# Local attention scores through DRAM bands, values weighed by rows of tokens on GpSimd and VectorE, from the third half-batch on

## The reference

```python
B, H, S, D = 4, 8, 576, 64; factor = 4; scale = 1 / sqrt(D)
# q, k, v pooled by the mean of 4 tokens: softmax attention over 144, each row repeated 4 times
out_up = repeat(softmax(scale * q_d @ k_d.T) @ v_d, factor)
# local attention: only keys with |i - j| < 4, so 7 of them
scores = where(abs(i - j) < factor, scale * q @ k.T, -1e9)
out_local = softmax(scores) @ v
x = (out_up + out_local) as (2304 tokens, 512)
h = x @ w1_in;  x = (h * sigmoid(h)) @ w1_out            # 512 -> 2048 -> 512
r = relu(x @ w2_in);  out = (s * r * r + b) @ w2_out     # 512 -> 2048 -> 512
```

## Time and profile before

| | |
|---|---|
| median of 3 runs | 978.97 us |
| profiled execution | 980.76 us, span 978.8 us |
| granted TensorE clock, mean | 0.997 |
| matmuls on the chain of waits | 93% of the span |
| VectorE, ScalarE, GpSimd busy | 46%, 38%, 36% |
| first layer, tile to tile | 69.3 us; 51.5 us for the last, without attention |

### The profile page before, as it was taken

How to read it: one execution, slowest core, us unless ns; L and a number is a source line. 1 busy time by engine, 2 the same in 40 slices (tenths; PEclk the granted TensorE clock), 3 DMA queues, 4 the chain that set the end, 5 groups by cost and what they waited for, 6 DMA issues and landing times.

```text
span 978.8 us, 17604 instructions
## 1 busy us (share of the span) xinstructions
PE 968.6 (99%) x6449; PEld 900.8 (92%) x6449; DVE 450.0 (46%) x1105; ACT 370.0 (38%) x1143; POOL 351.8 (36%) x366
## 2 busy tenths in 40 slices
PE   8999999999999999999999999999999999999998
PEld 8899999999999999999999998888888888888897
DVE  5577556565465555555554654224222322322232
...
DMA packets 71189, 60.64 MB, mean 62 GB/s; under 512 B 24272, under 2 KB 58576, under 8 KB 71120
## 3 DMA queue, kind: packets, MB, share of 16 engines
...
...
## 4 chain that ended last, share of the span: by engine, by line
PE 93%; DVE 4%; ACT 1%; issue 1%; DMA 1%; SPq 0%; POOL 0%; ACTq 0%; DVEq 0%
PE pH L599 20%; PE pY L614 20%; PE pH L541 19%; PE pY L546 18%; PE pO L484 4%; PE pS L441 3%; PE pO L480 2%; PE pO L457 2%; PE pS L444 2%; DVE w_in_hl L237 1%; PE pO L460 1%; DVE w_out_hl L237 1%; ACT w_in_hl L638 1%; DVE act L871 1%; PE pY L557 1%
## 5 line engine op out<-in xcount | busy, mean ns | idle before, releaser
L237 POOL TENSOR_TENSOR g_hl<-act,g_hl 128x288 fp32r<-128x288 f32 (+2 forms) x208 | 199.6, 960 | 602.4 <-ACT g_hl L638 602.4
L546 PE MATMUL pY<-g_hl,w_out_hl 128*128 128x288 f32 x1536 | 246.5, 300 | 0.4 <-POOL g_hl L237 0.4
L541 PE MATMUL pH<-x_hl,w_in_hl 128*128 128x288 f32 x1518 | 238.2, 301 | 2.8 <-issue 1.8
L541 PEld LDWEIGHTS pH<-x_hl,w_in_hl 128*128 128x128 f32 x1518 | 212.2, 190 | 3.2 <-issue 3.2
L546 PEld LDWEIGHTS pY<-g_hl,w_out_hl 128*128 128x128 f32 x1536 | 213.0, 188 | 0.6 <-POOL g_hl L237 0.6
L599 PE MATMUL pH<-x_hl,w_in_hl 128*128 128x512 f32 (+1 forms) x960 | 208.4, 368 | 0.0
L614 PE MATMUL pY<-w_out_hl,g_hl 128*128 128x512 f32 x864 | 207.8, 390 | 0.0
L599 PEld LDWEIGHTS pH<-x_hl,w_in_hl 128*128 128x128 f32 x960 | 169.0, 188 | 31.0
L614 PEld LDWEIGHTS pY<-w_out_hl,g_hl 128*128 128x128 f32 x864 | 161.2, 188 | 33.1 <-POOL g_hl L237 0.3
L638 ACT ACTIVATE g_hl<-act 128x288 fp32r<-128x288 f32 (+2 forms) x208 | 104.0, 500 | 213.8 <-DVE act L871 110.1
L992 DVE TENSOR_TENSOR act<-act 128x512 f32<-128x512 f32 (+1 forms) x80 | 55.5, 694 | 270.6 <-ACT act L793 270.6
...
## 6 DMA issues: line engine op xcount, KB each, us to landing
...
```

What stands on the lines that cost most here:

```text
L237: eng.tensor_tensor(lo, full, hi.bitcast(F32), ALU.subtract).then_inc(signal, 1)
L541: last = pe.matmul(pH[:, f % 2, 0:T1], w_in[:, wp, c, f * P:(f + 1) * P], x1[:, par, mp, c, :], start=c + n == 0, stop=c == C - 1 and n == 2)
L546: last = pe.matmul(pY[:, c, 0:T1], w_out[:, wp, f, c * P:(c + 1) * P], g_hl[:, f % RING, mp, 0:T1], start=f + n == 0, stop=f == NF - 1 and ...
```

## The change

Units 0 to 15 are done as before. From unit 16 on (`by_rows`), TensorE makes the scores as before, but ScalarE copies the three local blocks to SBUF in place of the exponentials, and SyncE stores them in DRAM (`store_band`) and reads only the 7 keys of each token back (`read_band`), so that a partition holds two heads of a block of 9 tokens: 4 pairs of heads by 32 blocks are 128 partitions. When a half's eight heads are there, one softmax is taken over the half, on VectorE and ScalarE: `row_shift`, `row_exps`, `row_normalise` (126 numbers a partition). For each row i of the 9 tokens a product of 896 numbers (2 heads, 7 keys, 64 features) is made by GpSimd, or by VectorE for i = 2, 5, 8 (`weigh`); VectorE sums over the keys (`sum_row`). TensorE transposes the rows in groups of three (`turn`), ScalarE moves them to `x_rows` (`place`), VectorE adds the pooled part (`x_add`), ScalarE rounds (`x_round`) and GpSimd subtracts (`x_low`). The values come in four loads a half (`load_windows`). The local transposes, local attends, masks and copies of these units go away.

To have the scores in time, a unit's scores are made seven units ahead: tile 1 works units 1 to 14 of its half and the next, two in each of slots 0 to 5; tiles 2 to 5 one a slot; tile 6 has one unit left. A loop pass is now tiles 2 and 3, then 4 and 5. Small edits: 20 short memsets for an edge mask ahead of `first_sums` on VectorE, a larger identity, buffers laid out anew, and the second layer's first weight loads behind the wait on `x1_ready`.

```diff
+TB = 9
+NB = HALF // TB
+NR = 2 * POOL - 1
+ROWS = TB + NR - 1
+BAND = KW + 1
+EDGES = 3
+NEW = 2 * H
+LEAD = 7
+UNITS = [(u + LEAD,) for u in range(H)]
+FIRST_UNITS = [(1, 2), (3, 4), (5, 6), (7, 8), (9, 10), (11, 12), (13,), (14,)]
+WEIGH = {2: (0, 1), 3: (2, 3), 4: (4, 5), 5: (6, 7), 6: (8,)}
+FIRST_WEIGH = {5: (0, 1, 2), 6: (3, 4, 5), 7: (6, 7, 8)}
+BY_VECTOR = (2, 5, 8)
+BY_POOL = tuple(i for i in range(TB) if i not in BY_VECTOR)
+GROUP = 3
+TURNS = {(4, 24): 0, (6, 24): 1, (7, 14): 2}
+FIRST_TURNS = {(6, 24): 0, (7, 12): 1, (7, 42): 2}
+ONE_UNIT, LAST_UNIT, FIRST_LAST_UNIT = (9, 15, 38), (3, 20, 38), (3, 18, 47)
+TWO_UNITS = (3, 7, 19), (27, 31, 43)
...
+    bands = nc.dram_tensor("score_bands", (2, H, HALF * BAND), F32).ap()
...
+        def by_rows(n):
+            return not (isinstance(n, int) and n < NEW)
...
+                def store_band(w):
+                    n, half, par, batch, u = w
+                    sp.wait_ge(exped, (NJ + 1) * (n + 1))
+                    sp.dma_start(bands[par, u].rearrange("(j x) -> j x", j=NJ)[:, 0:TQ * KW].rearrange(
+                        "j (q k) -> q j k", k=KW), s_sb).then_inc(bands_stored, 16)
+                def read_band(w):
+                    n, half, par, batch, u = w
+                    sp.wait_ge(bands_stored, 16 * (n - NEW) + 16)
+                    own = u % 2 * NR
+                    sp.dma_start(e_rows[u // 2 * NB:(u // 2 + 1) * NB, par, :, own:own + NR],
...
+                    if following:
+                        sp.wait_ge(rows_summed, TB * t)
+                        load_windows(following)
...
+                    if k < NJ and by_rows(n):
+                        return
...
+                    elif not by_rows(n):
...
+                def turn(t, g, w):
+                    if w:
+                        pe.wait_ge(pT_copied, w[0] + 1)
+                    else:
+                        pe.wait_ge(o_copied, H * (HALVES - 1))
+                    if g:
+                        pe.wait_ge(rows_placed, TB // GROUP * (t - 1) + g)
+                    pe.wait_ge(rows_summed, TB * (t - 1) + GROUP * (g + 1))
+                    for n in range(GROUP):
+                        last = pe.transpose(pO[:, n * P:(n + 1) * P], o_row[GROUP * g + n], ident[:])
+                    last.then_inc(rows_turned, 1)
...
+                    for v, (at_trans, at_scores, at_attend) in zip(now, places):
+                        if k == at_trans:
+                            trans_unit(unit(h, v - 1))
+                        if k == at_scores:
+                            score_unit(unit(h, v))
+                        if (u, k) in turns(t):
+                            turn(t, turns(t)[u, k], unit(h, v - 1))
+                        if k == at_attend and unit(h, v - 1):
+                            placed(t, u, k)
+                            attend_unit(unit(h, v - 1))
...
+                    if by_rows(n):
+                        if not (isinstance(n, int) and n == NEW):
+                            sc.wait_ge(bands_stored, 16 * (n - NEW))
+                        copy(s_sb, o.s_loc).then_inc(exped, NJ)
+                        return
...
+                def row_exps(t, h):
+                    sc.wait_ge(row_shifted, t)
+                    sc.activation(e_rows[:, h[1]], e_rows[:, h[1]], ACT.Exp, scale=SCALE).then_inc(row_exped, 1)
+                def place(t, h, g):
+                    sc.wait_ge(rows_turned, TB // GROUP * (t - 1) + g + 1)
+                    copy(x_rows[:, h[1], 1].rearrange("p c (b i) -> p i (c b)", i=TB)[:, GROUP * g:GROUP * (g + 1), :],
+                         pO[:, 0:GROUP * P].rearrange("p (i x) -> p i x", i=GROUP)).then_inc(rows_placed, 1)
+                def x_round(t, h, c):
+                    sc.wait_ge(x_added, C * (t - 1) + c + 1)
+                    copy(x1[:, h[1], 0, c, :], x_rows[:, h[1], 1, c, :]).then_inc(x_high, 1)
...
+                    tanh1(t, f)
+                    if last:
+                        place(t, h, here[0])
+                    g_high(L[0], t, f, 2, T1)
+                    if u == softmax_in(t):
+                        row_exps(t, h)
+                    if w := unit(h, now[0]):
+                        exps(w)
+                    if len(now) == 2:
+                        evacuate(unit(h, now[0] - 1)) if now[0] > 0 else None
+                    if not last:
+                        for g in here:
+                            place(t, h, g)
+                    if last and len(here) == 1:
+                        for c in range(C):
+                            x_round(t, h, c)
+                    for f in more:
+                        tanh1(t, f)
+                        g_high(L[0], t, f, 2, T1)
+                    if len(now) == 2:
+                        exps(unit(h, now[1]))
+                    if last and len(here) == 2:
+                        place(t, h, here[1])
+                        for c in range(C):
+                            x_round(t, h, c)
...
+                def weigh(t, i):
+                    n = TB * (t - 1) + i
+                    if i == BY_VECTOR[0]:
+                        ve.wait_ge(windows_loaded, 16 * C * t)
+                        ve.wait_ge(row_probs, t)
+                    ve.wait_ge(rows_summed, n - 1)
+                    ve.tensor_tensor(*weigh_operands(i), ALU.mult).then_inc(weighed_by_vector, 1)
+                def sum_row(t, i):
+                    if i in BY_VECTOR:
+                        weigh(t, i)
+                        ve.wait_ge(weighed_by_vector, len(BY_VECTOR) * (t - 1) + BY_VECTOR.index(i) + 1)
+                    else:
+                        ve.wait_ge(weighed_by_pool, len(BY_POOL) * (t - 1) + BY_POOL.index(i) + 1)
+                    if not (isinstance(t, int) and t == 1):
+                        ve.wait_ge(rows_turned, TB // GROUP * (t - 1))
+                    ve.tensor_reduce(o_row[i].rearrange("p (h d) -> p h d", h=2),
+                                     weighted[:, i % 2].rearrange("p (h r d) -> p h d r", h=2, r=NR), AX.X,
+                                     ALU.add).then_inc(rows_summed, 1)
...
+                def x_add(t, h, c):
+                    half, par, batch = h
+                    if c == 0:
+                        ve.wait_ge(rows_placed, TB // GROUP * t)
+                        ve.wait_ge(o_copied, H * half)
+                    x = x_rows[:, par, 1, c, :].rearrange("p (a r) -> p a r", r=POOL)
+                    ve.tensor_tensor(x, x, o_up(par, c).unsqueeze(2).to_broadcast([P, DQ, POOL]),
+                                     ALU.add).then_inc(x_added, 1)
...
+                    if w := unit(h, now[0] - 1):
+                        pT_copy(w)
+                    f, more = UPS[u][0], UPS[u][1:]
+                    gate1(t, f)
+                    if u == softmax_in(t):
+                        row_normalise(t, h)
+                    if last and len(groups(t, u)) == 1:
+                        for c in range(C):
+                            x_add(t, h, c)
+                    if w := unit(h, now[0]):
+                        maxima(w)
+                    for i in weighs[:1]:
+                        sum_row(t, i)
+                    if w := unit(h, now[0]):
+                        normalise(w)
+                    if len(now) == 2:
+                        pT_copy(unit(h, now[0]))
+                    for f in more:
+                        gate1(t, f)
+                    if len(now) == 2:
+                        maxima(unit(h, now[1]))
+                    for i in weighs[1:]:
+                        sum_row(t, i)
+                    if len(now) == 2:
+                        normalise(unit(h, now[1]))
+                    if u == softmax_in(t) - 1:
+                        row_shift(t, h)
+                    if last and len(groups(t, u)) == 2:
+                        for c in range(C):
+                            x_add(t, h, c)
...
+                def weigh(t, i):
+                    n = TB * (t - 1) + i
+                    if i == 0:
+                        gp.wait_ge(windows_loaded, 16 * C * t)
+                        gp.wait_ge(row_probs, t)
+                    if not (isinstance(n, int) and n < 2):
+                        gp.wait_ge(rows_summed, n - 1)
...
+                    if len(now) == 2:
+                        qk_sums(unit(h, now[1]))
+                    elif w := unit(h, now[0]):
+                        v_sums(w)
+                    for i in weighs[:1]:
+                        weigh(t, i)
+                    f, more = UPS[u][0], UPS[u][1:]
+                    g_low(L[0], t, f, T1)
+                    for i in weighs[1:]:
+                        weigh(t, i)
+                    if last and len(groups(t, u)) == 1:
+                        for c in range(C):
+                            x_low(t, h, c)
+                    for f in more:
+                        g_low(L[0], t, f, T1)
+                    if len(now) == 2:
```

(3 more changed lines are left out.)

322 lines of the change are left out of this document (266 added, 56 removed).

## The result

The changed kernel takes 1013.58 us (median of four runs, 1013.0 to 1015.92) against 979.62 of the kernel before beside it: a ratio of 1.035 (95% interval 1.033 to 1.0375), 34 us slower. The forecast was slower by 10 us, and its range ended at 1012. The profiled execution took 1015.92 us with a span of 1014.1.

A forecast was written before the change was run, and what follows sets the result against it. TensorE, 99% busy, was taken as the bound: 980.8 - 45.1 + 6.0 + 24.0 + 25.1 = 990.8 us, 10.0 slower, so a median of 989.0. The range went from 962 to 1012.

The forecast's parts named there:

- The work taken from TensorE (-39.1): TensorE: 48 units lose local transposes and attends, 45.1 us; 54 new transposes add 6.0; net 39.1 less if nothing waits.
- Prices: Times for 896 elements: GpSimd's product 2.1 us, VectorE's sum 1.1, VectorE's own product 1.1 to 1.3.
- forecast 6.0 a tile: Tiles 2 to 5: each waits 2.4 + 1.7 + 0.5 + 1.4 = 6.0 us, together 24.0.
- The scores' waits: Tiles 2 to 5: TensorE's scores wait for GpSimd's sums, 2.4 us in slot 3; late sums in slot 5 cost 0.5.
- The tile's end, 1.4: End of tiles 2 to 5: x_add, x_round and x_low end late for the next tile, 1.4 us.
- the sentence that the gate of the second up block is late but its down block comes only four blocks later: Tiles 2 to 5, slot 2 into 3: gate late behind a sum awaiting the first product; no wait was counted.
- The clock, 1.7 a tile: Tiles 2 to 5: TensorE's granted clock falls behind the scores' wait in slot 3, losing 1.7 us.
- At nothing: Items priced at zero: bands, SyncE queues, windows' loads, 20 memsets, tile 6's products; loop's branch stays one pass long.
- The sentence on SyncE's slack: Bands are wanted only slots later, so every SyncE queue has slack; windows' loads are wanted in the next slot 2.
- Tile 1: forecast 25.1: Tile 1: 5.5 us in slots 0 to 4, then 4.8, 3.1 and 10.0 in slots 5 to 7, one clock drop 1.7.
- The first rival, mostly slack: Reordering hides the products: tiles 2 to 5 wait 8.8 us, tile 1 15.6, a median of 964.3; chance 0.30.
- The rival of contention: GpSimd's products wait 1.0 for VectorE or delay it, 15 on the path; clock falls at tile ends, 8.5: 1012; chance 0.12.

The follow-up runs named there:

- the fastest kernel: The run with all orders, plus tile 1's maxima ahead of the gate, exponentials ahead of the high part, and row softmax in slot 4: 967.68 us.
- the run with all orders: Changed kernel with pooled sums first, row sums last, x_round and weight loads earlier, windows' loads moved, tile 1's first sums earlier: 977.61 us.
- the orders in place: Changed kernel with pooled sums ahead of products, row sums behind gates and normalisations, x_round ahead of exponentials, second layer's weight loads earlier: 985.28 us.

## Why the prediction was wrong in size

**The work taken from TensorE (-39.1) was nearly right.** Tiles without waits take 63.2 to 63.8, forecast 62.4 (by the prediction's own terms, eight slots of 7.72 and three turns of 0.34, it is 62.8). Tile 6 takes 55.2 for 53, with no wait inside it, and 54.6 in the fastest kernel: that floor was 1.6 to 2.2 short.

**Prices.** GpSimd's product was over by 0.4, VectorE's sum under by 0.66. The sum was scaled from rows that read densely; a stride of 64 elements had no row. In a tile of 2 to 5 nine sums make this 6 us more on VectorE, and six products 2.5 less on GpSimd. But the gate of the second up block waits for one product and one sum, 3.45 for a forecast 3.2: its lateness was foreseen, and the prices aren't what failed. VectorE's own products, forecast 1.1 to 1.3, took 1.85 in the mean, for the port.

**Tiles 2 to 5: forecast 6.0 a tile.** Tile 3 shows what each term was:

```profile
PE pO L614 <- ACT g_gap L836: 3.0, 3, 1.9
PE pS L587 <- POOL d_f L1440: 1.8, 2, 1.5
PE pH L737 <- POOL x_hl L320: 0.8, 1, 0.8
PE pY L742 <- POOL g_hl L320: 0.2, 1, 0.2
```

The scores' waits, forecast 2.4 and 0.5, are 1.5 and 0.3, right in place, a little too long. The tile's end, 1.4, is 0.8 to 1.7. Missing is the wait for the copy, 3.0 a tile and 12.4 in all: **this is the step that failed**, in the sentence that the gate of the second up block is late but its down block comes only four blocks later. I followed the gate to its down block, and not what stands behind it on ScalarE. With the row sums behind the gates the wait is gone, and the time is 14.0 less; the waits for `prob_d` halve with it (10.8 to 5.3), so the 14.0 isn't the copy's alone.

The clock, 1.7 a tile, is nothing in tiles 3 and 5: their windows have 1.00 behind waits of 1.5 and 1.9. Tile 2 starts in the last drop of tile 1, and tile 4 has two drops, 3.0 lost behind the stops at the branch and 1.7 behind its wait of 1.9 for the copy. The same wait cost the clock in one tile of four.

What a wait costs was also too low. Laid beside the same instructions of the run with all orders (272.3 to 335.6 us, no wait), TensorE in tile 3 is later by 3.6 behind the three waits for the copy (3.0 idle), by 2.2 behind the two of the scores (1.8) and by 1.3 behind the one for `x_hl` (0.8): the matmuls just behind a wait take longer, and TensorE is busy 65.1 for 63.0. Altogether the waits cost tile 3 8.2, forecast 6.0. So the 6.0 came near the 5.8 of idle time by luck: the copy at nothing and the clock at 1.7 half cancel. With 0.9 of the floor it makes 71.5 for 68.4.

**At nothing** stood the loop's branch and the windows' loads. The two meet: the second stop is 3.9, and 1.9 with the loads moved, which makes the tile 2.3 shorter (3.8 with the orders in place). The first stop was covered by the forecast for a tile's end alone; with `x_round` earlier it is 2.2 and has no releaser. The sentence on SyncE's slack asked when the windows are wanted, not what they run beside. The second layer's weight loads stand in no sentence of the prediction; GpSimd's `x1_ready` holds them for 47 us on SyncE, and with them and `x_round` earlier the last tile is 2.4 shorter.

**Tile 1: forecast 25.1, 95 long.** Waits of 18.6 were found where they were put: 4.0 in slots 0 to 4 (forecast 5.5; the terms given reach 5.46 and not 5.55, which makes it 4.6), 4.4 in slot 5 (4.8), 3.4 in slot 6 (3.1), 6.8 at the end (10.0). That is 4.8 less than forecast. The mis-sized term is the clock, one drop of 1.7. Its window has 0.91 over 101.6 us, which by the prediction's way of counting is 9.1 lost; the same 602 matmuls are busy 82.9 us, 78.1 in the fastest kernel, so that at least 4.8 of it is real. Half-speed stretches follow the waits of 4.4, 3.4, 2.4 and 3.6, not one.

**The sum.** By the tiles' lengths, forecast some 477 in all (3 under the sum's own 480, by rounding) and measured 503: 6.5 in tile 1, 10 in tiles 2, 3 and 5, 7 in tile 4, 3.4 in tiles 6 and 7. The first rival, mostly slack, was argued down with waits that come "from the order on the queues, not from the load". The reason was true, and it is also why its 964 can nearly be had: 967.7 was measured once the order fits.

The rival of contention, at 0.12, named 1012, the nearest value, but not for its reasons. It had GpSimd's products wait or make VectorE wait for 1.0 each, and the clock fall at every tile's end. GpSimd's 36 took 1.68 to 1.70 each, so none was held up; VectorE's 18 lost 0.77 each in the mean, 14 in all, and some 10 us less of VectorE took 8.5 off the time. At tiles' ends the clock fell behind tile 1 and at the branch, not behind the others.
